# Sink-window attention with two feed-forward layers: narrow reciprocals, later weight splits, and matrix products of zeros

## The reference

```
scores = scale * q @ k.T
keep = is_sink | in_window                     # n_sink = 4, window = 128
a = exp(where(keep, scores, -1e9) - rowmax)
a = a / (sum(a) + 1e-9)
x = a @ v                                      # 1536 x 512
h = x @ w_in;  x = max(0.01 * h, h) @ w_out    # layer 0
h = x @ w_in2; y = (h * sigmoid(h)) @ w_out2   # layer 1
```

## Time and profile before

| what | us |
|---|---|
| median of 3 runs (lowest, highest) | 690.28 (688.85, 691.59) |
| the profiled execution | 690.17 |
| its span, first to last instruction | 688.3 |
| PE busy | 635.7 (92%) |
| DVE busy | 320.0 (46%) |
| ACT busy | 298.9 (43%) |
| POOL busy | 111.1 (16%) |

### The profile page before, as it was taken

The page is one execution under the profiler, slowest core; times in us unless marked ns, Lnnn a source line. Parts: engine busy times, 40 slices in busy tenths (PEclk is TensorE's granted clock), DMA queues, the critical chain, the costliest instruction groups (busy, mean ns, idle before and its releaser), DMA issues.

```text
span 688.3 us, 8850 instructions
## 1 busy us (share of the span) xinstructions
PE 635.7 (92%) x3032; PEld 527.1 (77%) x3032; DVE 320.0 (46%) x644; ACT 298.9 (43%) x676; POOL 111.1 (16%) x141
## 2 busy tenths in 40 slices
PE   3675689998998999999999999999999999999997
PEld 3564577776776888888788888888888888888886
DVE  4899746676654567665322224333321232212232
ACT  5575545545554555653323336433332333223332
POOL 6465312423222233320000000000000000000000
PEclk9799799999999999999999999999999999999999
DMA  6552423343330213211002212223320112201101
GB/s 143 163 162 79 138 62 107 94 132 92 115 94 17 62 54 105 60 61 62 1 0 75 77 63 92 93 91 101 108 98 1 61 62 67 101 18 61 62 0 62
DMA packets 16940, 53.26 MB, mean 77 GB/s; under 512 B 2561, under 2 KB 2561, under 8 KB 16897
## 3 DMA queue, kind: packets, MB, share of 16 engines
q1 hardware_dynamic: 16896, 52.70, 24.7%
HBM read 49.55 MB, written 3.15 MB: 77 GB/s over the span
## 4 chain that ended last, share of the span: by engine, by line
PE 65%; issue 2%; DVE 1%; ACT 0%; POOLq 0%; POOL 0%; DVEq 0%; ACTq 0%
PE h_ps L774 31%; PE y_ps L800 31%; PE o_ps L740 1%; PE t_ps L708 1%; PE s_ps L695 1%; DVE win L578 0%; PE t_ps L718 0%; DVE g L589 0%; DVE pT L535 0%; DVE att L572 0%; PE o_ps L757 0%; POOLq L112 0%; PE t_ps L722 0%; POOL x L306 0%; DVE sum_eps L561 0%
## 5 line engine op out<-in xcount | busy, mean ns | idle before, releaser
L774 PE MATMUL h_ps<-x,win 128*128 128x512 f32 x1152 | 285.5, 395 | 6.6 <-POOL x L306 3.6
L774 PEld LDWEIGHTS h_ps<-x,win 128*128 128x128 f32 x1152 | 215.2, 190 | 50.4 <-issue 7.5
L454 ACT ACTIVATE g_f<-h_ps 128x512 f32<-128x512 f32 x96 | 57.2, 596 | 259.4 <-PE h_ps L774 259.3
L800 PE MATMUL y_ps<-g,wout 128*128 128x512 f32 x576 | 146.7, 395 | 1.2 <-PE o_ps L740 1.2
L800 PE MATMUL y_ps<-wout,g 128*128 128x512 f32 x576 | 138.2, 389 | 0.0
L584 DVE TENSOR_TENSOR wout<-w_raw,wout 128x512 fp32r<-128x512 f32 x64 | 47.2, 737 | 194.5 <-ACT wout L447 194.5
L800 PEld LDWEIGHTS y_ps<-wout,g 128*128 128x128 f32 x576 | 108.1, 188 | 22.5
L800 PEld LDWEIGHTS y_ps<-g,wout 128*128 128x128 f32 x576 | 103.7, 188 | 20.6 <-issue 1.9
L589 DVE TENSOR_TENSOR g<-g_f,g 128x512 fp32r<-128x512 f32 x96 | 66.2, 690 | 102.1 <-ACT g L456 102.0
L404 ACT ACTIVATE prob<-sm,neg_max 128x260 f32<-128x260 f32 (+1 forms) x96 | 46.9, 489 | 74.0 <-DVE neg_max L527 73.9
L456 ACT ACTIVATE g<-h_ps 128x512 fp32r<-128x512 f32 x96 | 56.9, 592 | 0.0
(11 more groups left out here) (71 smaller groups left out, 415.0 us busy)
## 6 DMA issues: line engine op xcount, KB each, us to landing
w_raw<-w SPq DMA_DIRECT2D x64, 512.0 KB, 3.3
qk_raw<-qk SPq DMA_DIRECT2D x48, 260.0 KB, 4.6
v_raw<-vt SPq DMA_DIRECT2D x12, 256.0 KB, 3.9
y<-qk_raw SPq DMA_DIRECT2D x12, 256.0 KB, 2.2
vs_raw<-vsink SPq DMA_DIRECT2D x8, 8.0 KB, 2.4
```

The costliest lines, as they stand in the source:

```text
L454: nc.scalar.activation(g_f32[:, F % 2, :], h_ps[:, :], func, alpha=slope)
L774: ins = mm(h_ps[:, :], win[:, split_slot[split_of[F]], wp, c * P:(c + 1) * P], x[:, xp, c, tokens(F)], start=(c == 0 and wp == HI and xp = ...
L800: ins = mm(y_ps[d][:, :], a[:, d * P:(d + 1) * P], r, start=(first and wp == HI and gp == HI), stop=(last and wp == LO))
```

## The change

- The row sums get a second column that holds 1e-9, set once. `invert_sums` adds the two columns with a reduction and takes the reciprocal of 4 values, not of 4 values repeated 64 times. POOL spreads them over 64 columns into a new tile `inv_wide` (`spread_inverse`, in slots 2e+2), which `turn_half` now waits for. On DVE `low_pair` stands ahead of `invert_sums`.
- In block 0 the input weights of step s are split in step s-2 (before: s-4), the output weights in s-1 (before: s-3).
- The scores of the head go round three banks (before: four). The bank set free, `y_ps[1]`, takes the products of a new tile of zeros, `filler`: 24 ahead of the first scores and 3 at the end of each slot of the head, each 128x128 by 128x512 in bfloat16. Nobody reads them.
- The sink values are loaded from ACT's queue at the very start and stacked by DVE before tile 0's k is split.
- In slot 19 PE does `hidden(0)`, then the slot's attention work, then `hidden(1)` and `project(0)`; ACT takes both hidden steps there.

```diff
         if s < FT:
-            at, at_out = s - 4, s - 3
+            at, at_out = s - 2, s - 1
...
-        row_sum = sb("row_sum", [P, 2, H // 2], F32)
+        row_sum = sb("row_sum", [P, 2, H // 2, 2], F32)
...
+        filler = sb("filler", [P, 2 * P], BF16)
...
         def s_bank(n):
-            if n < S_FOUR:
-                return (s_ps, h_ps, y_ps[0], y_ps[1])[n % 4]
-            return (s_ps, y_ps[0], y_ps[1])[n % 3] if n < S_THREE else s_ps
+            if n < S_THREE:
+                return (s_ps, h_ps, y_ps[0])[n % 3]
+            return s_ps if n >= S_TWO or n % 2 == 0 else y_ps[0]
...
+            def spread_inverse(e):
+                pool.wait_ge(norm_step, 2 * e + 3)
+                spread[0] = e + 1
+                wait(pool, t_written, job["half", e - 1] + 1 if e else 0)
+                nc.gpsimd.tensor_copy(inv_wide[:, :, :], row_inv[:, e % 2, :].unsqueeze(2).to_broadcast(
+                    [P, H // 2, D])).then_inc(inv_spread, 1)
...
+            for b in range(B):
+                for r in range(REP):
+                    n = H * NS
+                    act.dma_start(vs_raw[r * n:(r + 1) * n, b, :], vsink[b]).then_inc(vs_loaded, 16)
             high_qk(0, 0)
...
-                if not head:
+                if a == FS:
+                    exp(2 * a + 1)
+                    take_hidden(1)
+                elif not head:
...
             def invert_sums(e):
                 dve.wait_ge(exp_done, 4 * (e + 1))
-                wait(dve, t_written, job["half", e - 1] + 1 if e else 0)
-                nc.vector.tensor_scalar_add(sum_eps[:, :], row_sum[:, e % 2, :], 1e-9).then_inc(norm_step, 1)
-                dve.wait_ge(norm_step, 2 * e + 1)
-                nc.vector.reciprocal(row_inv[:, :, :],
-                                     sum_eps[:, :].unsqueeze(2).to_broadcast([P, H // 2, D])).then_inc(norm_step, 1)
+                wait(dve, inv_spread, e - 1)
+                nc.vector.tensor_reduce(sum_eps[:, :], row_sum[:, e % 2, :, :], mybir.AxisListType.X,
+                                        ALU.add).then_inc(norm_step, 1)
+                dve.wait_ge(norm_step, 2 * e + 2)
+                nc.vector.reciprocal(row_inv[:, e % 2, :], sum_eps[:, :]).then_inc(norm_step, 1)
...
             nc.vector.memset(prob_sink[:, :, :, :, :], 0.0).then_inc(zeroed, 1)
+            stack_sink_values()
...
+                if 2 <= a <= NPAIR + 1:
+                    low_pair(a - 2)
                 if a in inverted_in:
                     invert_sums(inverted_in[a])
-                if 2 <= a <= NPAIR + 1:
-                    low_pair(a - 2)
...
+            def fill(n):
+
+                for _ in range(n):
+                    mm(y_ps[1][:, :], filler[:, 0:P], filler[:, :].unsqueeze(1).to_broadcast([P, 2, 2 * P]),
+                       start=True, stop=True)
...
                 if a < FS:
+                    if a == 0:
+                        pe.wait_ge(filler_ready, 1)
+                        fill(24)
...
                         weigh_sinks(turned_in[a])
+                    fill(3)
+                    continue
+                if a == FS:
+                    scores(2 * a)
+                    hidden(0, 0)
+                    hidden(0, 1)
+                    turn_half(turned_in[a])
+                    scores(2 * a + 1)
+                    weigh_values(a - 2)
+                    turn_pair(a - 1)
+                    weigh_sinks(turned_in[a])
+                    hidden(1, 0)
+                    hidden(1, 1)
+                    project(0, 0)
+                    project(0, 1)
                     continue
```

More of the change, by code:

```diff
@@ L109, in sink_window_attention_two_ffn @@
     E_EARLY = 2 * TB
-    S_FOUR, S_THREE = 2 * FS - 2, 2 * FS
+    S_THREE, S_TWO = 2 * FS - 2, 2 * FS
     with ExitStack() as ctx:
@@ L145, in sink_window_attention_two_ffn @@
         prob_sink = sb("prob_sink", [P, 2, REP, H, NS], F32)
-        row_sum = sb("row_sum", [P, 2, H // 2], F32)
+        row_sum = sb("row_sum", [P, 2, H // 2, 2], F32)
         sum_eps = sb("sum_eps", [P, H // 2], F32)
-        row_inv = sb("row_inv", [P, H // 2, D], F32)
+        row_inv = sb("row_inv", [P, 2, H // 2], F32)
+        inv_wide = sb("inv_wide", [P, H // 2, D], F32)
         scale = sb("scale", [P, 2, P], F32)
@@ L186, in sink_window_attention_two_ffn @@
         zeroed = sem("zeroed")
+        filler_ready = sem("filler_ready")
         q_high, k_high = sem("q_high"), sem("k_high")
@@ L201, in sink_window_attention_two_ffn @@
         norm_step = sem("norm_step")
+        inv_spread = sem("inv_spread")
         scale_ready = sem("scale_ready")
@@ L272, in _ @@
                         load_v(T + 1)
[L273 to L277, removed]
                 if PAIRS <= a < 2 * PAIRS:
@@ L296, in const @@
                 ins.then_inc(const_step, 1)
-            gathered, v_done, x_done = [0], [0], [0]
+            gathered, v_done, x_done, spread = [0], [0], [0], [0]
+            def spread_inverse(e):
[4 more added lines that the diff above has]
+                    [P, H // 2, D])).then_inc(inv_spread, 1)
             def low_x(e):
@@ L316, in low_qk @@
                 wait(pool, x_ready, x_done[0])
+                wait(pool, inv_spread, spread[0])
                 wait(pool, k_ready, c if T else 0)
@@ L381, in _ @@
                     low_v(T, j // 2)
+                if u in inverted_in:
+                    spread_inverse(inverted_in[u])
                 if 0 < u <= NPAIR:
@@ L399, in exp @@
                 if n % 4 == 0:
-                    wait(act, norm_step, 2 * (e - 1))
+                    act.wait_ge(norm_step, 1 + 2 * max(e - 1, 0))
                 if u >= PR // 2:
@@ L405, in exp @@
                                      bias=neg_max[:, n % 4:n % 4 + 1],
-                                     accum_out=row_sum[:, e % 2, n % 4:n % 4 + 1]).then_inc(exp_done, 1)
+                                     accum_out=row_sum[:, e % 2, n % 4, 0:1]).then_inc(exp_done, 1)
             def high_qk(T, half):
@@ L629, in stack_sink_values @@
                                             ALU.mult).then_inc(vs_step, 1)
+            nc.vector.memset(filler[:, :], 0.0).then_inc(filler_ready, 1)
+            nc.vector.memset(row_sum[:, :, :, 1:2], 1e-9).then_inc(norm_step, 1)
             nc.vector.memset(prob_sink[:, :, :, :, :], 0.0).then_inc(zeroed, 1)
+            stack_sink_values()
             for half in range(2):
@@ L713, in turn_half @@
                 wait(pe, t_ready, freed(t_bank, k))
-                pe.wait_ge(norm_step, 2 * e + 2)
+                pe.wait_ge(inv_spread, e + 1)
                 bank_ = t_bank(k)
                 for c in range(2):
-                    src = row_inv[:, 2 * c:2 * c + 2, :].rearrange("p h d -> p (h d)")
+                    src = inv_wide[:, 2 * c:2 * c + 2, :].rearrange("p h d -> p (h d)")
                     ins = nc.tensor.transpose(bank_[:, c * P:(c + 1) * P], src, ident[:, :])
@@ L766, in hidden @@
                     if F == 0:
-                        pe.wait_ge(s_read, S_FOUR)
+                        pe.wait_ge(s_read, S_THREE)
                     if F % FT == 0 and layer == 0:
@@ L787, in project @@
                     if F == 0:
-                        pe.wait_ge(s_read, S_THREE)
+                        pe.wait_ge(s_read, S_TWO)
                         pe.wait_ge(t_ready, N_EARLY)
@@ L819, in _ @@
                     scores(2 * a)
-                if a == FS:
-                    hidden(0, 0)
-                    hidden(0, 1)
                 hidden(F + 1, 0)
```

2 lines of the change are left out of this document (removed).

## The result

The changed kernel takes 671.94 us (median of 4 runs, 670.45 to 675.19), the kernel before 689.57 us on the same chip (688.14 to 691.59). The ratio is 0.9749 with a 95% interval of 0.9704 to 0.9793: 2.5% faster, by 17.6 us. The forecast was 667.7, in a range of 657 to 681. The profiled execution took 672.19 us, its span 669.8 in place of 688.3.

The account below looks back on a forecast made before the run. The prediction took DVE, 90% busy, to bound the head and matmuls on PE the time after 97 us. Gains of 17.2 (head), 3.3 (slot 19) and 2.0 us (block 0) made 22.5: 690.2 to 667.7 us, range 657 to 681.

Parts of the forecast that it names:

- What bounded the head: Head, from slot 6 to the end of scale_half(7): DVE is the bound, busy 46.4 of 51.8 us, 90%.
- The prices of the narrow form: Head: reduction and reciprocal 0.16 us each, DVE wins 13.7 us; POOL's spreading copy 0.73 us each.
- rival B: Head: queues hold each other, POOL above all; 3.3 us a slot, 675.0 us in all; chance 0.20.
- The start of slot 6: Start of the head: slot 6 begins at 23.5 us (22.5 to 25) in place of 27.90.
- The 13 slots: Slots 6 to 18: PE's 33.8 us over 0.87 gives 39 us, 3.0 a slot, in place of 51.8.
- rival A: Head: tighter pipeline, engines at full, 33.8 us for the 13 slots; 659.8 us in all; chance 0.20.
- rival E: Head: DVE's time goes but the head hangs on loads; about 684 us in all; chance 0.05.
- Slot 19: First hidden(0) to first hidden(2) product: attention fills the gap before hidden(1); 15.3 falls to 12.0 us, 3.3 won.
- Block 0: Slots 20 to 33: less lag from reciprocals against late splits; 2 us won, between 5 lost and 6.4 won.
- rival C: Block 0: late splits make each of 14 slots wait 1.6 us, 22.4 lost; 692.1 us in all; chance 0.06.
- Rival D: Head: PE stays at the low clock, 5.2 us a slot, 68 for 13 slots; 696.7 us in all; chance 0.04.
- The expected mark: Sign for the forecast: granted clock at 1.00 from about 15 us to 200.

Follow-up runs that it names:

- e2: Changed kernel with DVE writing the wide 128x256 reciprocals itself again and without POOL's copy; the reduction stays: 691.65 us, ratio 1.0031.
- e6: Kernel before plus the narrow reciprocal alone (reduction, reciprocal of 4 values, POOL's copy): 671.12 us, ratio 0.9746.
- e1: Changed kernel without any products of zeros, nothing else altered: 671.86 us, ratio 0.9745.
- e4: Changed kernel with sink values loaded by SP in slot 1 and stacked by DVE in slot 4 again: 670.16 us, ratio 0.9719.
- e8: Changed kernel without products of zeros, sinks loaded in slot 3 and stacked in 7, first weights loaded in slots 12 to 15, splits at s-3 and s-2: 667.62 us.
- e9: Changed kernel without products of zeros, sinks stacked in slot 6, first weights loaded in slots 12 to 15, splits one slot earlier from step 4 on: 662.82 us.
- e5: Changed kernel with the first four weight loads in slots 12 to 15 in place of 4 to 7: 667.89 us, ratio 0.9696.
- e3: Changed kernel with the weight splits early again, at s-4 and s-3: 671.26 us, ratio 0.9732.
- e7: Changed kernel with weight splits one slot earlier, at s-3 and s-2: 669.65 us, ratio 0.9720.
- e10: Kernel before plus the narrow reciprocal and the first weight loads in slots 12 to 15: 668.61 us, ratio 0.9695.

## Why the prediction was right and wrong

**What bounded the head: right.** DVE at 90% was the bound, and e2 and e6 show from both sides that its reciprocal is what mattered. After it the busy times of the 13 slots are near those forecast: PE 34.98 (33.8), ACT 31.33 (31.2), DVE 31.25 (29.9), POOL 28.64 (32.1). For PE that is luck. I had 24.8 us of its own work and 9.0 of products of zeros; e1, without these, is still busy for 30.94 us in the same slots, so its own work was taken 6 us too low and the products, which add 4.0, 5 us too high.

**The prices of the narrow form: right for two, too high for one.** The reduction at 38.46 lasted 0.15 us and the reciprocal at 38.65 0.18 us, with POOL busy from 38.32 to 39.63; I had 0.16 each. They were not held as the addition of the earlier trace rows was; the splits with two SBUF inputs in slot 19 were, 1.26 and 1.81 us for 0.69. (The Trainium skill, GPSIMD Engine Reference, Key points, names VectorE instructions with two SBUF inputs as a case of contention with GpSimd. The splits agree; the reduction and the reciprocal have one input each.) POOL's copy took 0.40 us, not 0.73, and PE's waits from 28 to 67 us have no row for it; rival B did not happen. (Its 5.1 us for POOL in two slots add up to 4.8 by the rows that it names; 4.4 were measured.)

**The start of slot 6: the step that failed.** I had it at 23.5; it is 28.22, which is 4.7 of the 4.8 us by which the end of the head (67.27, not 62.5) was missed. The argument was that the last split for slot 6 stays at 21.61 because tile 1's second half was held up before as well. The order of time at the start of after:

```profile
0.74 4.16 ACTq L481 DMA_DIRECT2D vs_raw<-vsink  x8
...
9.05 1.08 DVE L628 CAST vs_hi<-vs_raw 128x128 fp32r<-128x128 f32 x1 [7.77 <-DMA vs_raw<-vsink]
...
11.60 1.29 DVE L642 TENSOR_TENSOR vs_st<-vs_part,block_of 128x512 fp32r<-128x512 f32 x2
12.81 1.32 DVE L654 TENSOR_TENSOR k_hl<-qk_raw,k_hl 128x528 fp32r<-128x528 f32 x2
13.54 2.39 SPq L243 DMA_DIRECT2D qk_raw<-qk  x4
...
18.96 1.28 POOL L327 TENSOR_TENSOR q_st<-qk_raw,q_st 64x512 fp32r<-64x512 f32 x1 [8.11 <-ACT q_st L424]
...
24.15 1.32 POOL L333 TENSOR_TENSOR k_hl<-qk_raw,k_hl 128x528 fp32r<-128x528 f32 x1
```

Two errors add up. Stacking began at 9.05 and not at 7.0, since the sink transfers took 4.5 us to land, not the 2.4 of the earlier trace rows, and the cast lasted 1.08 in place of 0.23: the first `k_hl` split ran at 12.81, 2.8 later than forecast. And I looked at the second half of tile 1 alone. In the kernel before, its first half is loaded as soon as the first `k_hl` is split, at 8.36, POOL is through with it at 16.50, and begins the second half at 18.95. Now both halves are issued together from 13.54 on, and at 18.96 POOL begins only the first of them: its last split for slot 6 ends at 24.15 + 1.32 = 25.47, and not at 21.61. These 3.9 us, and 0.9 more from there to the masked maximum (2.75 us in place of 1.9), are the missing 4.7. e4, which undoes the edit, gets only 1.9 of them back, since stacking must then stand somewhere else. With stacking behind slot 6's masked maxima, slot 6 does start at 23.4 (e8) and 23.6 (e9), the forecast's 23.5, and pays for it in the next slots.

**The 13 slots: the right number by a wrong sum.** 39.05 us against 39.0. But 2.7 of them are the hole for tile 2's loads, and without it the slots take 36.4 us (e5), 2.8 each. And the sum was PE's 33.8 us over 0.87, of which 9.0 were products of zeros: e1 takes those away and `hidden(0)` comes 0.23 us earlier, so PE's busy time was never the limit. The pipeline is tighter than I took it, as in rival A, and the load limit, rival E, was partly real. I had given them 0.20 and 0.05 as whole cases, and they came as parts that cancelled.

**Slot 19: mechanism right, size short.** `hidden(1)` lost its gap. 13.30 and not 12.0: the sum left no room for splits beside POOL, which last twice as long; 1.44 us of wait for `pT` come from that. The split of step 2, priced at 1.2 us, cost 0.66.

**Block 0: right net, wrong terms.** 2.2 us against 2. I had the reciprocals' lag and the late splits in one balance, and gave neither its size. Taken apart they are 7.9 won by the narrow reciprocal in the kernel before (e6) and 4.8 lost by the late splits (e3 against after); the 0.9 left over lies between e6 and e3 and was not taken apart. The first is larger than the 6.4 us of PE's idle time in that stretch, which I had named as the most that could be won: 105.2 us of busy PE were themselves not a floor, since e6 does the same products in 102.2. Of rival C's mechanism, 7 of 14 slots show it, at 0.76 us on average, not 1.6.

**Clock and products of zeros.** Rival D did not come: the level is 1.00 through the 13 slots, and e1 shows the same from 28 us on without the products. The expected mark, 1.00 from about 15 us on, was missed: after has 0.50 from 13.5 to 20 (above), although 24 products of zeros ran from 1.05 to 7.73. They took 6.7 us, between the 5.5 and 11 that I had for the two levels, so the clock did rise while they ran. Then PE stood for 5.83 us, until the first scores at 13.57, and these run at the lower level:

```profile
13.57 0.69 PE L718 MATMUL s_ps<-k_hl,q_st 128*128 128x128 f32 x2 [5.83 <-DVE k_hl L654]
```

**Sign and chances.** Faster was right. The range held the time, and what happened was parts of the forecast, of A and of E. That the sum fell on the narrow reciprocal and three other gains was wrong: e6 shows that the one edit carries it. The three score banks, the place of `low_pair` and the new order of slot 19 were not run alone; e3, which has them all and the early splits, is as fast as e6 (671.26 and 671.12).

## What to carry to other kernels

Compute a value once at its own size and let an idle engine spread it; on an in-order engine such an edit gives back its own time and the lag of what is queued behind it, in the head, where DVE was at its limit, and in slots 20 to 33 too, where it was busy for only two thirds of the time. Price each part of a bundle apart: here one edit won 17 us and the others came to nothing together, the late splits by moving 5 us of waiting from one stage to the next. When the bound of a stage goes, look at once at what its loads are queued behind: a transfer that nobody reads for ten slots was the next limit.

## What was not expected of the hardware

- *Busy time of PE is not a floor.* Slots 20 to 33 held 105.2 us of busy PE in before, 103.5 in after and 102.2 in e6, with 535 to 537 products and a granted clock of 1.00 in each. The products themselves are hardly shorter: a hidden product takes 397 ns on average in before and in e6, one of `project` 401 and 400, a value product 287 and 284. All durations added up make 123.2 and 122.0 us. So 1.2 of the 3.0 us are shorter products, and the rest is that they overlap more, since busy time counts an overlap once. What makes them overlap more was not tried.
- *The opening of `hidden(16)`.* Behind the same wait of 2.64 us for `x`, its 12 products take 4.58 us in after and 3.01 in e9 (the rows above). It is the clock. The first row is of after from its first such product on, the second of e9:

```profile
194.08:198.66 4.58, 4.58 (x14) 3.63 (x15) 0.00 (x0) 0.00 (x0) 0.00 (x0) 0.63 0.27 62
```

```profile
184.50:187.50 3.00, 3.00 (x14) 2.48 (x15) 0.00 (x0) 0.00 (x0) 0.00 (x0) 1.00 0.00 0
```

The granted clock falls to 0.50 just behind the wait in the traces of before, after, e1, e2, e3, e6, e7 and e10, where the 12 products take 4.4 to 5.4 us, and stays at 1.00 in e4, e5, e8 and e9, where they take 3.0; the rest of these four is 1.5 us shorter. PE had waited for the same 2.64 us in all but e2 (4.04). What decides is open, and one trace of each kernel can't tell whether it goes by kernel or by execution.

- *DVE beside POOL.* Held: the cast of 128x128 (1.08 for 0.23 us), the splits with two SBUF inputs (1.26 and 1.81 for 0.69). Not held: the reduction and the narrow reciprocal (0.15 and 0.18).
- *Small transfers on a second queue.* Eight issues of 8 KB took ACT 4.16 us and landed 4.5 us after issue (the median), against 3.83 and 2.4 on SP later in the kernel before.
